# An attention + two-MoE kernel: transposed q and k from the host, 32-row windows, unrolled pair loop, five dummy transposes per pair

## The reference

```python
q_d, k_d, v_d = means over groups of 4 positions      # 144 positions
out_up = repeat(softmax(q_d @ k_d.T / 8) @ v_d, 4)     # down-sampled, full
mask = abs(i - j) < 4                                  # local: 7 keys per query
out_local = softmax(where(mask, q @ k.T / 8, -1e9)) @ v
x = (out_up + out_local).transpose(0, 2, 1, 3).reshape(1152, 512)
```

## Time and profile before

| | us |
|---|---|
| median of 3 runs | 708.74 |
| the profiled execution, its own time | 708.72 |
| its span, first to last instruction | 706.6 |
| TensorE busy | 676.7 (96%) |
| VectorE / ScalarE / GpSimd busy | 241.7 / 187.9 / 173.5 |
| TensorE's last tile of attention (`values` of pair 7) ends | about 102.5 |
| TensorE without a gap from | 111.3 |
| last TensorE work | about 702.2 |

### The profile page before, as it was taken

The page is one execution under the profiler, slowest core; times in us unless marked ns, Lnnn a source line. Parts: engine busy times, 40 slices in busy tenths (PEclk is TensorE's granted clock), DMA queues, the critical chain, the costliest instruction groups (busy, mean ns, idle before and its releaser), DMA issues.

```text
span 706.6 us, 11146 instructions
## 1 busy us (share of the span) xinstructions
PE 676.7 (96%) x3958; PEld 622.3 (88%) x3958; DVE 241.7 (34%) x376; ACT 187.9 (27%) x399; POOL 173.5 (25%) x121
## 2 busy tenths in 40 slices
PE   6768889999999999999999999999999999999997
PEld 5546679999999999998989899999999998989896
DVE  6988968753222322221221212121212121212211
ACT  4765873322111213343101142111241111101010
POOL 5836467660000004546000063000261000000000
PEclk9986989999999999999999999999999999999999
DMA  9454523430000002324100033000040000001001
GB/s 183 102 107 97 136 77 129 143 116 1 1 1 1 0 0 89 119 90 142 36 0 0 1 120 119 0 0 0 30 148 0 0 0 0 0 0 45 21 23 45
DMA packets 66870, 37.48 MB, mean 53 GB/s; under 512 B 32672, under 2 KB 59552, under 8 KB 66848
## 3 DMA queue, kind: packets, MB, share of 16 engines
q1 hardware_dynamic: 66848, 37.19, 18.7%
HBM read 34.82 MB, written 2.36 MB: 53 GB/s over the span
## 4 chain that ended last, share of the span: by engine, by line
PE 88%; DVE 4%; SPq 3%; issue 2%; DMA 1%; ACT 1%; DVEq 0%; POOL 0%; ACTq 0%; POOLq 0%
PE ps L874 42%; PE ps L940 28%; PE ps L924 14%; SPq L278 2%; DMA k_raw<-k 1%; SPq L258 1%; PE ps L789 1%; PE ps L856 1%; PE ps L777 1%; PE ps L841 1%; DVE g_hi L713 1%; PE ps L885 1%; DVE pl L669 0%; DVE kz L434 0%; DVE mx L643 0%
## 5 line engine op out<-in xcount | busy, mean ns | idle before, releaser
L733 DVE SCALAR_TENSOR_TENSOR g_lo<-ps,g_hi 128x384 fp32r<-128x384 f32 x96 | 53.5, 558 | 270.7 <-ACT g_hi L568 270.7
L568 ACT ACTIVATE g_hi<-ps 128x384 fp32r<-128x384 f32 x96 | 47.1, 491 | 293.5 <-PE ps L874 293.5
L397 POOL TENSOR_TENSOR wa_lo<-w_raw,wa_hi 128x1024 f32 (+1 forms) x24 | 57.4, 2395 | 214.8 <-ACT wa_hi L440 214.8
L874 PE MATMUL ps<-x_hi,wa_hi 128*128 (+1 forms) x288 | 97.6, 339 | 2.2 <-issue 2.2
L874 PE MATMUL ps<-x_hi,wa_lo 128*128 (+1 forms) x288 | 97.4, 338 | 0.0
L874 PE MATMUL ps<-x_lo,wa_hi 128*128 (+1 forms) x288 | 97.2, 338 | 0.0
L874 PE MATMUL ps<-x_hi,wb_hi 128*128 (+1 forms) x288 | 96.9, 336 | 0.0
L874 PE MATMUL ps<-x_lo,wb_hi 128*128 (+1 forms) x288 | 96.9, 336 | 0.0
L874 PE MATMUL ps<-x_hi,wb_lo 128*128 (+1 forms) x288 | 96.8, 336 | 0.0
L397 POOL TENSOR_TENSOR wb_lo<-w_raw,wb_hi 128x1024 f32 x24 | 57.7, 2408 | 106.7 <-ACT wb_hi L440 106.4
L713 DVE CAST g_hi<-g_act 128x384 fp32r<-128x384 f32 x48 | 42.7, 889 | 111.3 <-ACT g_act L563 111.3
(11 more groups left out here) (99 smaller groups left out, 1018.5 us busy)
## 6 DMA issues: line engine op xcount, KB each, us to landing
w_raw<-moe_w SPq DMA_DIRECT2D x64, 256.0 KB, 2.8
w_raw<-moe_w_in SPq DMA_DIRECT2D x16, 256.0 KB, 2.9
w_raw<-moe_w_out SPq DMA_DIRECT2D x16, 256.0 KB, 3.0
q_raw<-q SPq DMA_DIRECT2D x16, 144.0 KB, 3.6
k_raw<-k SPq DMA_DIRECT2D x16, 144.0 KB, 3.7
v_raw<-v SPq DMA_DIRECT2D x8, 288.0 KB
out<-o_acc SPq DMA_DIRECT2D x9, 256.0 KB, 2.0
v_win<-v SPq DMA_DIRECT2D x56, 35.0 KB
```

What stands on the lines that cost most here:

```text
L397: pool.tensor_tensor(lo[:, at, :].rearrange("p o n -> p (o n)"), w_raw[:, s, :], hi[:, at, :].rearrange("p o n -> p (o n)").bitcast(F32), ...
L568: act.activation(g_hi[:, f % GB, :], ps[:, HB + f % 4, 0:NB], ACT.Relu).then_inc(relu_done, 1)
L733: dve.scalar_tensor_tensor(out=g_lo[:, f % GB, :], in0=ps[:, HB + f % 4, 0:NB], scalar=0.0, in1=g_hi[:, f % GB, :].bitcast(F32), op0=ALU.m ...
L874: ins = pe.matmul(dst, w[:, f % HALF, c], x[:, kt, at], start=(kt == 0 and i == 0), stop=(kt == KT - 1 and i == 2))
```

## The change

Everything up to the split of x is rewritten; the MoE tiles are the same instructions. In words:

- The host transposes q and k for each pair, pads k by 3 positions, lays out v in 18 windows of 48 rows and in the down-sampling order, and packs each weight unit into one contiguous block. Transfers per pair: one for q and k (593 KB), one for v (295 KB), two for the windows (221 KB each); one for a unit.
- `turn_q`, `turn_k` and their copies are gone. Windows have 32 queries and 38 keys: 18 windows, one matmul for each head and window in `scores` (36 for a pair, 38 columns) and in `values` (36, 32 columns). Scores stay in PSUM through mask, maximum, subtraction, exponential and sum, in one buffer: `scores(n)` waits for `pl_ready` of pair n-1. Both heads' probabilities are transposed together: 5 transposes for a pair, not 10.
- The pair loop is unrolled and one stage shorter; VectorE now scales the down-sampled probabilities (`norm_down`).
- x of the second batch (pairs 4 to 7) is split after attention, beside the first MoE block.
- `warm(5)` stands in `values` of each pair, `warm` of 3, 6, 5 and 3 in steps 0 and 1.

```diff
-GQ = 64
+GQ = 32
+HS = 64
+ROWS = 48
...
+        EARLY = {1: 0, 2: 1, 3: 2, N: 3}
...
@@ SP
+            def load_qk(n):
+                if n >= 2:
+                    sp.wait_ge(s_full, n - 1)
+                    sp.wait_ge(qkd_ready, 2 * n - 2)
+                sp.dma_start(qk_raw[:, n % 2, :], qk[n]).then_inc(qk_in[n % 2], 16)
...
@@ GpSimd
+                pool.tensor_tensor(q2[:, :], qv[:, :, 0], qv[:, :, 1], ALU.add).then_inc(qk2_done, 1)
+                pool.wait_ge(qk2_done, max(2 * n, 1))
+                if n >= 1:
+                    pool.wait_ge(sd_full, n)
...
+            def step(s):
+                stage(s, down_qk)
+                stage(s - 1, down_v)
+                if s - 4 in range(XHALF):
+                    x_low(s - 4)
+                if s in EARLY:
+                    u = EARLY[s]
+                    low_unit(u + 1, slice(u, u + 1), areas[0], u % RAW)
...
             low_units(0, areas[0], 2)
+            for n in range(XHALF, N):
+                x_low(n)
             low_units(HALF, areas[1])
...
@@ ScalarE
             def split_hi(u):
-                act.wait_ge(raw_in[u % RAW], 32 * (u // RAW + 1))
+                act.wait_ge(raw_in[u % RAW], 16 * (u // RAW + 1))
                 if u == HALF:
-                    act.wait_ge(xlo_done, N + 1)
+                    act.wait_ge(xlo_done, N)
...
+            def step(s):
+                if s == N + 1:
+                    hidden1(0, 0)
+                stage(s - 2, evac_p1)
+                stage(s - 2, evac_pd)
+                stage(s - 1, evac_p0)
+                stage(s, exp_local)
+                stage(s, exp_down)
...
+                stage(s - 2, evac_up)
+                if s - 4 in range(XHALF):
+                    x_high(s - 4)
+                if s in EARLY:
+                    split_hi(EARLY[s])
...
@@ VectorE
+                dve.tensor_tensor(local_scores(0, LC), local_scores(0, LC), m, ALU.add).then_inc(dve_step, 1)
...
+            def step(s):
+                stage(s, mask_scores)
+                stage(s, max_local)
+                stage(s, sub_max)
+                stage(s, max_down)
+                stage(s, norm_local)
+                stage(s, norm_down)
+                stage(s - 2, final)
+                if s == N:
                     hidden1(0, 0)
...
@@ TensorE
+                for g in range(G):
+                    t, c = g // QP, g % QP
+                    at = t * W
+                    for h in range(2):
+                        rows = slice(D * h, D * h + D)
+                        ins = pe.matmul(ps[GQ * c:GQ * c + GQ, SLB + h, at:at + W],
+                                        qk_raw[rows, par, GQ * g:GQ * g + GQ],
+                                        qk_raw[rows, par, S + GQ * g:S + GQ * g + W], start=True, stop=True)
...
+            def values(n):
+                par = n % 2
+                pe.wait_ge(p0_out, n + 1)
+                pe.wait_ge(p1_out, n + 1)
+                pe.wait_ge(vw_in[par], 32 * (n // 2 + 1))
+                if n >= 1:
+                    pe.wait_ge(xf_done, n)
+                warm(WARM[5])
+                for turn_over in range(2):
+                    for i in range(G // 2):
+                        for h in range(2):
+                            bank = (turn_over + h) % 2
...
+            WARM = (8, 3, 6, 5, 3, 5)
+
+            def step(s):
+                if s == N + 1:
+                    in1(0, 1)
+                stage(s, scores)
+                if s == 0:
+                    warm(WARM[1])
+                stage(s - 1, turn_p0)
+                stage(s, scores_down)
+                if s < 2:
+                    warm(WARM[2 + s])
+                stage(s - 2, values)
+                if s == N:
+                    pe.wait_ge(xlo_done, XHALF)
                     pe.wait_ge(expd_done, 4 * N)
                     in1(0, 0)
+                stage(s - 1, turn_p1)
```

More of the change, by code:

```diff
@@ L173, in program, with stage, x_of @@
         block = ctx.enter_context(nc.Block())
[L181 to L229, removed]
+        def stage(n, do):
+            if 0 <= n < N:
+                do(n)
+        EARLY = {1: 0, 2: 1, 3: 2, N: 3}
+        XHALF = N // 2
+        def x_of(x, n):
+            return x[:, n % KT, (n // KT) * S:(n // KT) * S + S]
         def tile1(blk, f):
@@ L262, in load_v @@
[L262 to L292, removed]
@@ L301, in _ @@
+            load_qk(0)
+            for s in range(N + 1):
+                step(s)
+            with sp.Fori(2, (FT1 + E * FT2) // RAW) as i:
                 for s in range(RAW):
@@ L574, in end1 @@
                     copy(x_hi[:, j, bass.ds(blk * NB, NB)], ps[:, ACCB + j, 0:NB]).then_inc(x2hi_done, 1)
-            steps(act, step, 4)
+            act.wait_ge(band_set, 2)
+            for c in range(2):
+                copy(*window_mask(c)).then_inc(mask_set, 1)
+            for s in range(N + 2):
+                step(s)
             AHEAD = len(EARLY)
@@ L582, in _ @@
                     split_hi(f + AHEAD)
+                if f + XHALF < N:
+                    x_high(f + XHALF)
             end1(0)
@@ L716, in hidden1 @@
                                   ALU.subtract).then_inc(g_ready, 1)
-            steps(dve, step, 3)
+            dve.wait_ge(band_set, 2)
+            for c in range(2, QP):
+                dve.tensor_copy(*window_mask(c)).then_inc(mask_set, 1)
+            down_k(0)
+            for s in range(N + 2):
+                step(s)
             dve.wait_ge(pr_in, 16)
@@ L819, in scores, with warm, turn_local @@
-            def scores(duo, par):
-                for bank in range(2):
-                    pe.wait_ge(tp_free[bank], tp_before_qk(duo, par) + 2)
-                if late(duo, par, 1):
-                    pe.wait_ge(masked, 2 * pair(duo, par))
+            def warm(count):
+                for _ in range(count):
+                    pe.transpose(ps[:, OUTB, 0:P], ident[:, :], ident[:, :])
+            def turn_local(n, bank, at, t):
+                return pe.transpose(ps[0:PW, TB + bank, at:at + P],
+                                    pl[:, n % 2, t, :, :].rearrange("p h j -> p (h j)")[:, 0:PW], ident[:, :])
@@ new lines, in turn_down, with turn_p0 @@
+            def turn_down(n, bank, at, i):
+                s, h, half = i // 4, (i // 2) % 2, i % 2
+                return pe.transpose(ps[0:HQ, TB + bank, at:at + HQ],
+                                    pd[:, n % 2, 2 * h + half, s * HQ:(s + 1) * HQ], ident[0:HQ, 0:HQ])
+            def turn_p0(n):
+                pe.wait_ge(pl_ready, n + 1)
+                if n == 0:
+                    pe.wait_ge(zeroed, 3)
+                if n >= 1:
+                    pe.wait_ge(pd_out, n)
+                for t in range(GT - 1):
+                    ins = turn_local(n, 0, t * P, t)
+                ins.then_inc(p0_turned, 1)
```

638 lines of the change are left out of this document (278 added, 360 removed).

## The result

The changed kernel takes 721.38 us (median of four runs, 720.99 to 721.69); the kernel before took 708.97 on the same chip. The ratio is 1.0182, with a 95% interval of 1.0148 to 1.0215: slower, 28 us above the predicted 693 and outside the range. The profiled execution took 721.57 us, with a span of 719.7.

The account below looks back on a forecast made before the run. Attention's pairs, through VectorE and k transfers, bound the kernel ahead of a solid MoE block; values(7) ending at 87.4, plus 8.0 and 595.3, gave a span of 690.7 and 692.8 us (predicted 693), range 679 to 705.

Parts of the forecast that it names:

- What bounds the kernel: Before the MoE block, the chain goes through k transfers and VectorE; pairs 10.7 us each, so the gain is a shorter pair.
- the fixed parts: After attention: values(7) to out1(0, 1) 8.0 us, then 595.3 us to the span's end; 2.1 us outside the span.
- VectorE's chain: Per pair, mask to pl_ready: 6.3 us after the step starts, below TensorE's 7.8, so not bounding alone; sets steps 0 and 1.
- GpSimd late, the loop: Attention pairs: down_qk behind low_unit or x_low makes TensorE idle; pairs of 10.2 us in steps 2 to 4, 8.8 in 5 to 7.
- rival 2: Attention pairs: TensorE's clock stays low, transposes and scores_down double; +9 to +14 us, 702 to 707; chance 0.12.
- The sum: Whole kernel: values of pair 7 end at 87.4 us, plus 8.0 and 595.3 give a span of 690.7, time 692.8 us.
- five dummies a pair: In front of each pair's values: five dummy transposes, 0.67 us, counted against the clock staying low.
- Small records: TensorE's scores and values per pair: 72 records each at 28 ns, 2.0 us for either group.
- Rival 4: Attention's 1,152 tiny records are dear: 42 ns each loses all 15.9 us of gain, 50 ns gives 718; chance 0.07.
- The deferred split: First MoE block: unit 8 ready at about +22 us after pair 7's values, wanted at +27; nothing added, bounds 0 and 7 us.
- rival 3: First MoE block: split_hi(8) waits for the last x_low, hidden1(5) behind it; unit 8 late gives 698 to 700; chance 0.06.
- Transfers: Attention pairs: SP's queue leaves the chain, 1.33 MB per pair takes 5.7 us, hidden; the k wait of 4.12 us goes.

Follow-up runs that it names:

- e2: Changed kernel with GpSimd down-sampling q and k of the next pair before it splits a weight unit or x: 696.7 us, ratio 0.986 to the kernel before.
- e1: Changed kernel without the five dummy transposes in front of each pair's values: 711.6 us, ratio 1.007 to the kernel before.
- e4: Changed kernel, local value products with 32 of v's 64 stationary columns, half the local output left out: 704.4 us, ratio 0.996 to the kernel before.
- e10: e3 with two neighbouring windows sharing one stationary operand in local values, 20 matmuls for 36, result partly wrong: 683.1 us, ratio 0.964 to the kernel before.
- e12: e3 with ScalarE's split_hi of units 8 and above issued one tile later: 690.3 us, ratio 0.973 to the kernel before.
- e3: Changed kernel without the pairs' dummies and with down-sampling one pair ahead: 689.8 us, ratio 0.976 to the kernel before.
- e5: Changed kernel with seven more dummy transposes where TensorE waits ahead of scores_down, steps 2 to 7: 708.1 us, ratio 0.999 to the kernel before.
- e6: Changed kernel with one float32 matmul of 512 columns where TensorE waits ahead of scores_down: 708.1 us, ratio 1.002 to the kernel before.
- e9: Kernel before with only its inputs changed: q, k and v laid out by the host, turn_q, turn_k and copies gone: 702.2 us, ratio 0.994.

## Why the prediction was wrong

**What bounds the kernel, and the fixed parts: right.** From `values(7)` to out1(0, 1) it took 7.8 us (forecast 8.0), and the block behind kept its length but for the stall's 3.5 us.

**VectorE's chain: right.** Its first pairs come 6.2 and 5.3 us apart (forecast 6.3), each of its operations on 380 elements takes 0.55 us, and VectorE has 1% of the chain.

**GpSimd late, the loop: right in its mechanism.** The q addition starts right behind `x_low`, `scores_down` waits for `kd`; e2 opens the loop and wins 23 us (by the ratios) to 25 us (by the medians) against the changed kernel. At full clock the loop would have been as forecast: with this trace's own full-clock distances for `scores_down` (0.65), dummies, values and down-sampled values, 12.33 and 13.66 us become 8.9 and 10.2, an estimate from these rows, against the forecast's 8.8 and 10.2. But rival 2 took what a low clock adds as "partly hidden behind GpSimd". It is in series: what TensorE takes for `scores_down`, dummies, values and down-sampled values delays `evac_up`, hence GpSimd, hence TensorE.

**The failed step: the clock, rival 2.** The sum took every TensorE term of the loop at clock 1.00; the low clock held 0.12 of the chance and was priced at +9 to +14 us. At 0.50 for the whole loop, values cost 2.0 us a pair more than forecast, dummies 0.6, down-sampled values 0.56 and `scores_down` 0.4: 3.5 us in series, with pairs 2 to 7 and the steps behind them. I had counted only transposes and `scores_down` as twice as long. The sum of `values(7)`: 113.1 against 87.4, which is 25.7, is made of -1.9 (early start of scores(2)), +21.6 (six pairs) and about +6 (steps 8 and 9, where in1(0, 0) took 4.03 us, not 2.1). That five dummies a pair hold the clock, which I took from the earlier trace rows, fell with e1. That the first 13 transposes were followed by a faster pace shows that the clock can rise then, not that five of them a pair suffice.

**Small records: near for values, far off for scores.** 28 ns was forecast for both. Values at full clock cost 30.7 ns, scores 10.6 ns (last section), together 3.0 us a pair against 4.0; as scores don't lie on the loop, the 1 us that they save gave nothing. The price isn't one of moving columns: in e4 and e10 the values records go by their stationary columns, with 64 of them 31 to 33 ns at 2.4 GHz and 55 at 1.2. Rival 4's 718 has nearly the right time for another reason: a values record did cost more than its 42 ns, through the clock.

**The deferred split, rival 3: right as a mechanism, missed in the chance.** I took the gap to be covered with a margin of 5 us. That margin was TensorE's for unit 8, and unit 8 was not what came late: hidden1(5), queued behind its `split_hi`, is needed sooner. It cost 3.5 us in the changed kernel; e12 removes 3.8 from e3.

**Transfers: right.** No wait of SP is on the chain (0%), and the k wait of 4.12 us is gone.

**What stays open.** Why the clock is low. Idle time plays a part (e5 and e6, some 12 us back, and e2). It isn't the whole: in e3 the clock falls inside a pair with no gap, over scores and turns, and rises in values; e10, with fewer, wider value matmuls, has 0.72 and 0.87. Nor do only small matmuls run slow: the 384-column records of out1(0, 0), right behind `values(7)` in the changed kernel and without a gap before them, start 0.32 us apart in place of 0.17 from 113.7 us on, at a clock of 0.50. What the granted clock answers to was not isolated, and windows of 32 rows alone in the kernel before weren't tried. Where the clock is low through all pairs the times agree (0.7 us between the four runs of the changed kernel, 2.1 between e1's ten); where it comes and goes they spread by up to 12 us.

**The fastest version with a right result** is e3 (0.976 of the kernel before) or e12 (0.973), which the times don't tell apart. Between e9's 0.994 and e3 lie about 1.8%, for windows, order and unrolling together; they weren't separated.

## What to carry to other kernels

Work out a pair's loop through the engines' queues with TensorE at both of its clock levels: a loop in which TensorE waits once per turn and works in small pieces can sit at 1.2 GHz for its whole length (here 89 us), and what TensorE does on it then takes up to twice as long. Before adding dummies look whether they lie on the loop, and try the reordering that closes the wait first: here it gave 23 us. With dummies in front of values each of the three kernels in which they were tried was slower than without; only work put exactly where TensorE idled won something (12 to 13 us), and less than the reordering. When a small matmul is priced, look for a row with as many stationary columns, and the same placement in the array.

## What the runs showed of the hardware

The 72 records of `scores` (32 stationary, 38 moving columns) in the changed kernel, at full and at half clock:

```profile
9.88 0.83 PE L707 MATMUL ps<-qk_raw 64*32 64x38 f32 x72 [1.52 <-DVE pl L565]
10.64 0.65 PE L664 MATMUL ps<-ident,pl 128*102 128x128 f32 x4
...
57.84 1.08 PE L707 MATMUL ps<-qk_raw 64*32 64x38 f32 x72
58.85 1.09 PE L664 MATMUL ps<-ident,pl 128*102 128x128 f32 x4
```

0.76 us for 72, or 10.6 ns each, well under the floor of about 25 ns of the Trainium skill (TensorE: Matmul & The Clock Gate, section Back-to-back issue gap) that the prediction weighed. At half clock they take 1.01 us, or 14 ns each, where e4's values records, also with 32 stationary columns, take 29. So stationary columns alone don't give the price. What differs is the number of rows (64 against 38) and the placement: by the kernel's slices the records of `scores` go in turn to two halves of the input partitions and four groups of output partitions, those of values to two halves of either, each half always with its own. Which of the two is the cause was not tested.

VectorE's tiny operation reading PSUM took 0.17 us each time, in e3 also beside a GpSimd instruction (at 38.70, GpSimd's began at 38.67), where the one between SBUF operands had waited 1.16 us for GpSimd.

The recorded clock is not enough by itself; the pace of like records has to go with it. It is recorded as 1.00 at the very start of the kernel before, where transposes run at 234 ns, the pace of the lower level (252 ns in the changed kernel's pairs, 128 at full clock). And one of the four runs of the changed kernel has a recorded mean of 1.000, with 720.99 us, where the other three have 0.932 to 0.934.
